# A second halved square per chunk, its low part as the third pass, T3 ahead of y, and the split of x1 shared with ScalarE

## The chip, the cores and the metric

The kernel runs on one core of one Trainium2 chip. The metric is the device time of one execution in microseconds. TensorE does matmuls, VectorE, ScalarE and GpSimd work elementwise, each with its own queue of instructions in a fixed order; semaphores tie the queues together. In profile rows they are PE (and PEld for its weight loads), DVE, ACT and POOL.

## The reference

```python
# attention over pooled keys, with k = v, then two MLPs, all fp32
kv_flat = kv.reshape(B, H//4, 4, W//4, 4, C).mean(axis=(2, 4)).reshape(B, -1, C) @ w_sr
a = softmax(q @ kv_flat.T / sqrt(C));  x = a @ kv_flat          # 12288 tokens x 128
x = (relu(x @ w_in1) ** 2) @ w_out1                             # d_ff 2048
h = x @ w_in2
P = a[0] + a[1]*h + a[2]*h**2 + a[3]*h**3
Q = 1 + |b[0]|*|h| + |b[1]|*h**2
out = (P / (Q + 1e-6)) @ w_out2
```

## The kernel before

Everything is kept transposed: 128 features on the partitions, tokens along the free dimension. Stage A (the first 300 us) is the attention and leaves X. Stage B, the other 1200 us, is both MLPs, in 24 chunks (NCH) of 512 tokens (T), each with 16 tiles of 128 hidden features (NF); 384 tiles (NB) in all.

Precision: an fp32 matmul is one instruction, shown as two records. Where a cheaper way is used, an operand is split into a rounded fp32r part ("h", high) and the rest ("l", low), and three fp32r passes (h.h, h.l, l.h) replace the fp32 matmul: in1 and in2, the first layers of both MLPs, always run so, through the helper three().

Each engine's program is a Python loop over steps s, unrolled; there is no planner. In step s:
- TensorE: in2(s - 19), then in1(s), then out2(s - 23), then out1(s - 2). in2 and in1 are the first layers, out2 and out1 the second ones, which add into one PSUM bank over the 16 tiles of a chunk. LAG = 19 is the distance of the second MLP behind the first.
- ScalarE, in this order: osb (the output copy of a finished chunk) in column 7, x2h and x2f (the high part and a full copy of the first MLP's result) in column 2, g1h (the high part of a halved square) and the square of tile s - 1 where it is ScalarE's, then for tile s - 19 the abs u and t1 = a3 h + a2 (tb), an hcb copy of h in column 10, ln of the denominator of tile s - 20, relu of tile s, and exp of tile s - 20, which gives r = 1/Q.
- GpSimd: in column 2 x2l = x2f - x2h; v = |b1| u + |b0| and w = v u of tile s - 19, with the T2 product of that tile between them in column 10 (T2_COL = 7, by_pool); then, if s is odd, the square of tile s, and g1l for a halved tile.
- VectorE: y = (t3 + a0) r of tile s - 21, T3 = (t2 + a1) h of tile s - 20, E (in place over r, from w) of tile s - 21, T2 = t1 h of tile s - 19, G2 of tile s - 21, the result that out2 reads.

"Column" here is s modulo 16. Squares of even tiles are ScalarE's, those of odd tiles GpSimd's; in chunk 0 ScalarE and VectorE make all of them. SPLIT_COLS = (13,) says which square of a chunk is "halved": ScalarE makes its high part g1h, GpSimd its low part g1l = g1 - g1h, and out1 runs three fp32r passes for that tile in place of one fp32 matmul.

Each chunk of X is split too, into x1h and x1l, by GpSimd: x1_high and x1_low in the loop from L388 on, in column 5 of the chunk before (chunks 2 to 23; the first two are split in stage A). in1 of the chunk's first tile waits for it (x1_rdy).

Rings: four PSUM banks for h (H2_RING), so in2(t) waits for G2 of tile t - 4; two for the first MLP (in1(t) waits for relu of tile t - 2). exp writes over h, so it waits for T3. out1 of a chunk's first tile waits for x2f of the chunk before, in2 of a chunk's first tile for x2l (L909). The DMA queue does nothing here but one output a chunk.

The only lines that order VectorE's work around the change are these:

```python
            for s in range(TAIL_S):
                t = s - LAG - 2      # y, waits r_rdy
...
                t = s - LAG - 1      # T3, waits t2_rdy or t2p_rdy
...
                t = s - LAG - 2      # E
...
                t = s - LAG          # T2, waits t1_rdy
...
                t = s - LAG - 2      # G2
```

Of the kernel before, what the change touches and what calls it, by code (L numbers as in the profile page):

```python
# [30 lines left out]
def build_program(nc, qT, kvT, w_sr, w_in1, w_out1, w_in2, w_out2, coef_a, coef_b, outT):  # L31
# [35 lines left out]
    with ExitStack() as ctx:  # L67
# [91 lines left out]
        sqh_rdy, sql_rdy = sem("sqh_rdy"), sem("sql_rdy")  # L159
        x2f_rdy, x2l0_rdy = sem("x2f_rdy"), sem("x2l0_rdy")  # L160
        wo1h_rdy, wo1_rdy, g1h_rdy, g1l_rdy = map(sem, ("wo1h_rdy", "wo1_rdy", "g1h_rdy", "g1l_rdy"))
        hc_rdy, t2p_rdy = sem("hc_rdy"), sem("t2p_rdy")
        o_out = [sem("o_out0"), sem("o_out1")]
        wout1_in = sem("wout1_in")
# [39 lines left out]

            return t < NF or t % 2 == 0

        SPLIT_COLS = (13,)

        def halved(t):

# [76 lines left out]
        def _(pool):  # L287
# [61 lines left out]

            def x1_low(c):  # L350

                pool.wait_ge(x1h_rdy, c + 1)
                nc.gpsimd.tensor_tensor(x1l[:, c % 2, :], X[:, c * T:(c + 1) * T], x1h[:, c % 2, :].bitcast(F32),
                                        ALU.subtract).then_inc(x1_rdy, 1)

# [30 lines left out]
            pool.wait_ge(babs_rdy, 1)  # L386

            for s in range(STEPS):  # L388
                if s % NF == 5 and 1 <= s // NF < NCH - 1:
                    x1_high(s // NF + 1)  # L390
                    x1_low(s // NF + 1)
                t = s - 3
                if chunk_end(t) and t > NF:
                    c = t // NF
                    pool.wait_ge(x2h_rdy, c + 1)
                    pool.wait_ge(x2f_rdy, c)
                    nc.gpsimd.tensor_tensor(x2l[:, c % 2, :], x2f[:, c % 2, :], x2h[:, c % 2, :].bitcast(F32),  # L397
                                            ALU.subtract).then_inc(x2_rdy, 1)
                t = s - LAG
                if in_b(t):  # L400
                    w = wb[:, t % W_RING, :]
                    u = ub[:, t % U_RING, :]
                    pool.wait_ge(u_rdy, t + 1)
                    nc.gpsimd.tensor_scalar(w, u, babs[:, 1:2], babs[:, 0:1], ALU.mult, ALU.add).then_inc(v_rdy, 1)  # L404
                    if by_pool(t):
                        n = pool_t2(t)
                        p = tb[:, t % T_RING, :]
                        pool.wait_ge(t1_rdy, t + 1)
                        pool.wait_ge(hc_rdy, n + 1)
                        nc.gpsimd.tensor_tensor(p, p, hcb[:, n % HC_RING, :], ALU.mult).then_inc(t2p_rdy, 1)  # L410
                    pool.wait_ge(v_rdy, t + 1)
                    nc.gpsimd.tensor_tensor(w, w, u, ALU.mult).then_inc(w_rdy, 1)  # L412
                t = s
                if in_b(t) and not on_act(t):
                    r = r1[:, t % R_RING, :]
                    pool.wait_ge(r1_rdy, t + 1)
                    need(pool, g1_used, t - G_RING + 1)
                    nc.gpsimd.tensor_tensor(g1[:, t % G_RING, :], r, r, ALU.mult).then_inc(sqp_rdy, 1)  # L418
                    if halved(t):
                        n = halves(t)  # L420
                        pool.wait_ge(sqh_rdy, n + 1)
                        pool.wait_ge(sqp_rdy, squares_pool(t))
                        nc.gpsimd.tensor_tensor(g1l[:, n % 2, :], g1[:, t % G_RING, :], g1h[:, n % 2, :].bitcast(F32),
                                                ALU.subtract).then_inc(sql_rdy, 1)
# [3 lines left out]
        def _(act):  # L428
# [78 lines left out]
            for s in range(STEPS):  # L507
# [35 lines left out]
                if s == NF + 1:  # L543
                    act.wait_ge(g1_used, NF)
                    nc.scalar.activation(x2h[:, 0, :], ACC1, ACT.Identity).then_inc(x2h_rdy, 1)

                t = s - LAG
                if in_b(t):
# [40 lines left out]
        def _(dve):  # L589
# [129 lines left out]
            dve.wait_ge(x2h_rdy, 1)  # L719
            nc.vector.tensor_tensor(x2l[:, 0, :], ACC1, x2h[:, 0, :].bitcast(F32), ALU.subtract).then_inc(x2l0_rdy, 1)  # L720

            for s in range(TAIL_S):
                t = s - LAG - 2
                if in_b(t):
                    y, r = tb[:, t % T_RING, :], h2(t)
                    dve.wait_ge(r_rdy, t + 1)
                    nc.vector.scalar_tensor_tensor(out=y, in0=y, scalar=ca[:, 0:1], in1=r,  # L727
                                                   op0=ALU.add, op1=ALU.mult).then_inc(y_rdy, 1)
                t = s - LAG - 1
                if in_b(t):  # L730
                    p = tb[:, t % T_RING, :]
                    if by_pool(t):
                        dve.wait_ge(t2p_rdy, pool_t2(t) + 1)
                    else:
                        dve.wait_ge(t2_rdy, t + 1 - pool_t2(t + 1))
                    nc.vector.scalar_tensor_tensor(out=p, in0=p, scalar=ca[:, 1:2], in1=h2(t),  # L736
                                                   op0=ALU.add, op1=ALU.mult).then_inc(t3_rdy, 1)
                t = s - LAG - 2
                if in_b(t):
                    r = h2(t)  # L740
                    nc.vector.scalar_tensor_tensor(out=r, in0=wb[:, t % W_RING, :], scalar=Q_ONE, in1=r,  # L741
                                                   op0=ALU.add, op1=ALU.mult).then_inc(e_rdy, 1)
                t = s - LAG
                if in_b(t) and not by_pool(t):
                    p = tb[:, t % T_RING, :]
                    dve.wait_ge(t1_rdy, t + 1)
                    nc.vector.tensor_tensor(p, p, h2(t), ALU.mult).then_inc(t2_rdy, 1)  # L747
                t = s - LAG - 2
                if in_b(t):
                    y = tb[:, t % T_RING, :]  # L750
                    dve.wait_ge(y_rdy, t + 1)
                    dve.wait_ge(e_rdy, t + 1)
                    nc.vector.scalar_tensor_tensor(out=y, in0=h2(t), scalar=-2.0, in1=y,  # L753
                                                   op0=ALU.add, op1=ALU.mult).then_inc(g2_rdy, 1)

            for s in range(TAIL_S, STEPS):
                t = s - LAG - 2
                if in_b(t):
                    y, r = tb[:, t % T_RING, :], h2(t)
                    dve.wait_ge(r_rdy, t + 1)  # L760
                    nc.vector.scalar_tensor_tensor(out=y, in0=y, scalar=ca[:, 0:1], in1=r,
                                                   op0=ALU.add, op1=ALU.mult).then_inc(y_rdy, 1)
                t = s - LAG - 1
                if in_b(t):
                    p = tb[:, t % T_RING, :]
                    if by_pool(t):
                        dve.wait_ge(t2p_rdy, pool_t2(t) + 1)
                    else:
                        dve.wait_ge(t2_rdy, t + 1 - pool_t2(t + 1))
                    nc.vector.scalar_tensor_tensor(out=p, in0=p, scalar=ca[:, 1:2], in1=h2(t),  # L770
                                                   op0=ALU.add, op1=ALU.mult).then_inc(t3_rdy, 1)
                t = s - LAG
                if in_b(t) and not by_pool(t):
                    p = tb[:, t % T_RING, :]
# [20 lines left out]
        def _(pe):  # L795
# [106 lines left out]
            def in2(t):  # L902

                if in_b(t):
                    c, f = t // NF, t % NF * P
                    if t == 0:
                        pe.wait_ge(wl_rdy, W_PARTS)
                    if t % NF == 0:
                        pe.wait_ge(*((x2l0_rdy, 1) if c == 0 else (x2_rdy, c)))  # L909
                    if t < WIDE + H2_RING:  # L910
                        need(pe, g2_rdy, t - H2_RING + 1)
                    elif t < WIDE + TAIL_RING:
                        pe.wait_ge(r1_rdy, NB)
                    else:
                        pe.wait_ge(g2_rdy, t - TAIL_RING + 1)
                    three(h2(t), win2h[:, f:f + P], win2l[:, f:f + P],
                          x2h[:, c % 2, :], x2l[:, c % 2, :]).then_inc(h2_rdy, 1)

            def in1(t):

# [26 lines left out]
            def out1(t):  # L947

                if in_b(t):
# [13 lines left out]
                    elif halved(t):  # L963
                        n = halves(t)
                        pe.wait_ge(sqh_rdy, n + 1)
                        pe.wait_ge(sql_rdy, n + 1)
                        three(ACC1, wo1h[:, f, :], wo1l[:, f, :], g1h[:, n % 2, :], g1l[:, n % 2, :],
                              start=(f == 0), stop=(f == NF - 1)).then_inc(g1_used, 1)
                    else:
                        if on_act(t):  # L970
                            pe.wait_ge(sqa_rdy, squares_act(t))
                        else:
                            pe.wait_ge(sqp_rdy, squares_pool(t))
                        mm(ACC1, wout1[:, f, :], g1[:, t % G_RING, :], start=(f == 0), stop=(f == NF - 1))\  # L974
                            .then_inc(g1_used, 1)
# [51 lines left out]
```

## Time and profile before

| | us |
|---|---|
| median of 3 runs | 1517.82 (1517.7 to 1518.0) |
| the profiled execution | 1517.89 |
| its span, first to last instruction | 1515.9 |
| TensorE busy | 1483.7 (98%) |
| VectorE busy | 1445.2 (95%) |
| ScalarE busy | 1378.8 (91%) |
| GpSimd busy | 1248.3 (82%) |

The granted clock of TensorE is 1.00 of full speed over the span. Busy times are unions of records, from an instruction's start to its end; since a next instruction may start before the last one's record ends, they say less than start times do. Matmul ends are modelled, and a matmul behind an fp32 one has its start shown early, so steps are best measured from the first x1h pass of a step (in1) to the next.

### The profile page before, as it was taken

To read this page: it belongs to the slowest core of one execution; us is meant where nothing else is said; L and a number is where in the kernel's file an instruction comes from. 1 tells how busy PE (TensorE), PEld (TensorE's weight loads), DVE (VectorE), ACT (ScalarE), POOL (GpSimd) and SP (SyncE) were. 2 spreads that over 40 slices of the span, in tenths; PEclk is the share of its full clock that TensorE was granted. 3 is DMA by queue.
4 is the path that set the end of the run, shared out by engine and by line. 5 is a ranking of instruction groups with operands and counts; after the bars stand their busy time and mean duration, and the time that the engine had idled before them with its cause. 6 is when DMAs were issued, how large, how long until landed. Compare 5 with 4: busy or idle time off the path is not lost.

```text
span 1515.9 us, 20584 instructions
## 1 busy us (share of the span) xinstructions
PE 1483.7 (98%) x5576; PEld 991.1 (65%) x5576; DVE 1445.2 (95%) x2549; ACT 1378.8 (91%) x2672; POOL 1248.3 (82%) x1225
## 2 busy tenths in 40 slices
PE   5999999999999999999999999999999999999988
PEld 4999999765666666666666666666666666666655
DVE  7888888889999999999999999999999999999998
ACT  3777777689999999999999999999999999999997
POOL 4544445359999999999999999999999999999897
PEclk9999999999999999999999999999999999999999
DMA  6200001000000000000000000000000000000000
GB/s 224 84 21 28 21 27 43 1 1 1 8 8 8 1 8 8 8 8 1 7 8 8 0 8 8 8 1 8 7 8 1 8 8 8 8 1 8 8 8 7
DMA packets 11518, 24.21 MB, mean 16 GB/s; under 512 B 1440, under 2 KB 2336, under 8 KB 11168
## 3 DMA queue, kind: packets, MB, share of 16 engines
q1 hardware_dynamic: 11424, 23.14, 4.5%
q8 instruction: 36, 0.59, 0.2%
q14 instruction: 58, 0.48, 0.1%
HBM read 16.85 MB, written 6.29 MB: 15 GB/s over the span
## 4 chain that ended last, share of the span: by engine, by line
PE 88%; DVE 5%; ACT 2%; POOL 2%; issue 1%; DMA 1%; SPq 0%; POOLq 0%; ACTq 0%; DVEq 0%
PE psum L937 19%; PE psum L974 18%; PE psum L801 11%; PE psum L800 11%; PE psum L802 11%; PE psum L889 6%; PE psum L852 6%; PE psum L874 4%; DVE tb L727 1%; DVE tb L736 1%; DVE tb L753 1%; DVE g1h L713 1%; DVE psum L741 1%; POOL tb L410 1%; DMA X<-kvT 1%
## 5 line engine op out<-in xcount | busy, mean ns | idle before, releaser
L412 POOL TENSOR_TENSOR wb<-wb,ub 128x512 f32<-128x512 f32 x384 | 496.4, 1293 | 29.4
L937 PE MATMUL psum<-tb,wout 128*128 128x512 f32 x736 | 375.8, 592 | 2.5 <-DVE tb L785 2.3
L974 PE MATMUL psum<-g,wout 128*128 128x512 f32 x690 | 352.4, 592 | 0.2 <-ACT x2f L528 0.2
L404 POOL TENSOR_SCALAR wb<-ub,babs 128x512 f32<-128x512 f32 x384 | 296.0, 771 | 35.5 <-ACT ub L550 30.3
L800 PE MATMUL psum<-x2h,win2h 128*128 128x512 f32 x384 | 283.3, 738 | 2.6 <-POOL x2l L397 2.5
L727 DVE SCALAR_TENSOR_TENSOR tb<-tb,ca,psum 128x512 f32<-128x512 f32 x364 | 267.8, 736 | 4.6 <-ACT psum L584 4.5
L736 DVE SCALAR_TENSOR_TENSOR tb<-tb,ca,psum 128x512 f32<-128x512 f32 x365 | 269.6, 739 | 0.0
L551 ACT ACTIVATE tb<-psum,ca 128x512 f32<-128x512 f32 x384 | 267.1, 696 | 0.0
L550 ACT ACTIVATE ub<-psum 128x512 f32<-128x512 f32 x384 | 233.0, 607 | 23.5 <-PE psum L802 23.5
L568 ACT ACTIVATE lnb<-wb 128x512 f32<-128x512 f32 x384 | 248.3, 647 | 5.2 <-POOL wb L412 4.8
L753 DVE SCALAR_TENSOR_TENSOR tb<-psum,tb 128x512 f32<-128x512 f32 x364 | 248.1, 682 | 2.6
L741 DVE SCALAR_TENSOR_TENSOR psum<-wb,psum 128x512 f32<-128x512 f32 x364 | 249.5, 685 | 0.0
L584 ACT ACTIVATE psum<-lnb 128x512 f32<-128x512 f32 x384 | 240.1, 625 | 2.6 <-DVE tb L770 0.6
L974 PEld LDWEIGHTS psum<-g,wout 128*128 128x128 f32 x690 | 130.9, 190 | 163.7 <-issue 162.0
L578 ACT ACTIVATE r<-psum 128x512 f32<-128x512 f32 x384 | 234.9, 612 | 2.4 <-PE psum L802 0.3
L747 DVE TENSOR_TENSOR tb<-tb,psum 128x512 f32<-128x512 f32 x343 | 232.5, 678 | 4.0 <-ACT tb L551 4.0
L418 POOL TENSOR_TENSOR g<-r 128x512 f32<-128x512 f32 x184 | 191.9, 1043 | 33.2 <-ACT r L578 33.2
L334 POOL TENSOR_SCALAR pnorm<-prob,stat 128x768 f32<-128x768 f32 x96 | 87.3, 909 | 127.8 <-DVE stat L637 122.0
L937 PEld LDWEIGHTS psum<-tb,wout 128*128 128x128 f32 x736 | 138.4, 188 | 36.4 <-DVE tb L785 3.8
L801 PE MATMUL psum<-x1l,win1h 128*128 128x512 f32 x384 | 153.0, 398 | 0.0
L801 PE MATMUL psum<-x2l,win2h 128*128 128x512 f32 x384 | 152.9, 398 | 0.0
L800 PE MATMUL psum<-x1h,win1h 128*128 128x512 f32 x384 | 151.9, 396 | 0.0
(109 smaller groups left out, 2506.6 us busy)
## 6 DMA issues: line engine op xcount, KB each, us to landing
qraw<-qT SPq DMA_DIRECT2D x23, 256.0 KB, 2.6
outT<-osb SPq DMA_DIRECT2D x23, 256.0 KB, 2.0
X<-kvT SPq DMA_DIRECT2D x15, 384.0 KB, 7.7
wraw<-w_in SPq DMA_DIRECT2D x2, 1024.0 KB, 8.3
X<-kvT SPq DMA_DIRECT2D x2, 192.0 KB, 10.5
outT<-osb SPq DMA_DIRECT2D x2, 128.0 KB, 1.8
qraw<-qT SPq DMA_DIRECT2D x1, 192.0 KB, 10.2
wsr<-w_sr SPq DMA_DIRECT2D x1, 64.0 KB, 1.8
```

Source lines behind the costliest of these rows:

```text
L404: nc.gpsimd.tensor_scalar(w, u, babs[:, 1:2], babs[:, 0:1], ALU.mult, ALU.add).then_inc(v_rdy, 1)
L412: nc.gpsimd.tensor_tensor(w, w, u, ALU.mult).then_inc(w_rdy, 1)
L551: nc.scalar.activation(tb[:, t % T_RING, :], h2(t), ACT.Identity, bias=ca[:, 2:3], scale=a3).then_inc(t1_rdy, 1)
L568: nc.scalar.activation(lnb[:, t % LN_RING, :], wb[:, t % W_RING, :], ACT.Ln, bias=Q_ONE).then_inc(ln_rdy, 1)
L727: nc.vector.scalar_tensor_tensor(out=y, in0=y, scalar=ca[:, 0:1], in1=r, op0=ALU.add, op1=ALU.mult).then_inc(y_rdy, 1)
L736: nc.vector.scalar_tensor_tensor(out=p, in0=p, scalar=ca[:, 1:2], in1=h2(t), op0=ALU.add, op1=ALU.mult).then_inc(t3_rdy, 1)
L741: nc.vector.scalar_tensor_tensor(out=r, in0=wb[:, t % W_RING, :], scalar=Q_ONE, in1=r, op0=ALU.add, op1=ALU.mult).then_inc(e_rdy, 1)
L753: nc.vector.scalar_tensor_tensor(out=y, in0=h2(t), scalar=-2.0, in1=y, op0=ALU.add, op1=ALU.mult).then_inc(g2_rdy, 1)
L800: mm(out, lh, rh, start=start, stop=False)
L801: mm(out, lh, rl, start=False, stop=False)
L937: mm(ACC2, wout2[:, f, :], tb[:, t % T_RING, :], start=(f == 0), stop=(f == NF - 1))\
L974: mm(ACC1, wout1[:, f, :], g1[:, t % G_RING, :], start=(f == 0), stop=(f == NF - 1))\
```

## The change

Four things:
- SPLIT_COLS is (5, 13): the square of tile 5 of each chunk from chunk 1 on is halved as well. ScalarE makes one more g1h (in column 6), GpSimd one more g1l (in column 5), TensorE three fp32r passes in place of an fp32 matmul.
- The order of passes in in2 and in out1 of halved tiles: the two passes that need the high part alone come first, and the wait for the low part stands only in front of the third. (In the code above L908 to L917 and L964 to L968.)
- VectorE's loop runs T3 (tile s - 20) before y (tile s - 21), except in steps whose T3 needs GpSimd's T2 product (column 11). In the steps from TAIL_S on the order is as before.
- x1's high part for chunks 2 to 23 is made by ScalarE in column 8, ahead of that step's abs; GpSimd's x1_low moves from column 5 to column 10, ahead of that step's v, and waits for the new semaphore.

```diff
-        SPLIT_COLS = (13,)
+        SPLIT_COLS = (5, 13)
...
             def x1_low(c):
-                pool.wait_ge(x1h_rdy, c + 1)
+                pool.wait_ge(*((x1h_rdy, c + 1) if c < 2 else (x1ha_rdy, c - 1)))
...
             for s in range(STEPS):
-                if s % NF == 5 and 1 <= s // NF < NCH - 1:
-                    x1_high(s // NF + 1)
+                if s % NF == 10 and 1 <= s // NF < NCH - 1:
                     x1_low(s // NF + 1)
...
+                if s % NF == 8 and 1 <= s // NF < NCH - 1:
+                    c = s // NF + 1
+                    act.wait_ge(x_rdy, c + 1)
+                    need(act, h1_rdy, (c - 1) * NF)
+                    nc.scalar.activation(x1h[:, c % 2, :], X[:, c * T:(c + 1) * T], ACT.Identity).then_inc(x1ha_rdy, 1)
...
+            for s in range(TAIL_S):
+                if by_pool(s - LAG - 1):
+                    make_y(s - LAG - 2)
+                    make_t3(s - LAG - 1)
+                else:
+                    make_t3(s - LAG - 1)
+                    make_y(s - LAG - 2)
...
                     if t % NF == 0:
-                        pe.wait_ge(*((x2l0_rdy, 1) if c == 0 else (x2_rdy, c)))
+                        pe.wait_ge(x2h_rdy, c + 1)
...
-                    three(h2(t), win2h[:, f:f + P], win2l[:, f:f + P],
-                          x2h[:, c % 2, :], x2l[:, c % 2, :]).then_inc(h2_rdy, 1)
+                    mm(h2(t), win2h[:, f:f + P], x2h[:, c % 2, :], start=True, stop=False)
+                    mm(h2(t), win2l[:, f:f + P], x2h[:, c % 2, :], start=False, stop=False)
+                    if t % NF == 0:
+                        pe.wait_ge(*((x2l0_rdy, 1) if c == 0 else (x2_rdy, c)))
+                    mm(h2(t), win2h[:, f:f + P], x2l[:, c % 2, :], start=False, stop=True).then_inc(h2_rdy, 1)
...
                         pe.wait_ge(sqh_rdy, n + 1)
+                        mm(ACC1, wo1h[:, f, :], g1h[:, n % 2, :], start=(f == 0), stop=False)
+                        mm(ACC1, wo1l[:, f, :], g1h[:, n % 2, :], start=False, stop=False)
                         pe.wait_ge(sql_rdy, n + 1)
-                        three(ACC1, wo1h[:, f, :], wo1l[:, f, :], g1h[:, n % 2, :], g1l[:, n % 2, :],
-                              start=(f == 0), stop=(f == NF - 1)).then_inc(g1_used, 1)
+                        mm(ACC1, wo1h[:, f, :], g1l[:, n % 2, :], start=False, stop=(f == NF - 1)).then_inc(g1_used, 1)
```

make_y and make_t3 hold the two instructions of the loop before, word for word.

## Rows read from the trace of the kernel before

**Rows 1.** The page: shares of the chain that ended last, by engine
```profile
PE 88%; DVE 5%; ACT 2%; POOL 2%; issue 1%; DMA 1%; SPq 0%; POOLq 0%; ACTq 0%; DVEq 0%
```

**Rows 2.** Windows: PE, PEld, DVE, ACT, POOL busy us, clock, DMA, GB/s
```profile
1000.00:1200.00 200.00, 200.00 (x649) 122.22 (x648) 198.81 (x320) 195.97 (x376) 187.11 (x182) 1.00 0.02 6
```

**Rows 3.** Timeline of PE: start us, us, line, op, out<-in; first x1h passes
```profile
703.78 0.39 PE L800 MATMUL psum<-x1h,win1h 128*128 128x512 f32 x1
...
706.73 0.40 PE L800 MATMUL psum<-x1h,win1h 128*128 128x512 f32 x1
...
756.38 0.40 PE L800 MATMUL psum<-x1h,win1h 128*128 128x512 f32 x1
```

**Rows 4.** Timeline of ACT in a stretch where it has a backlog
```profile
335.06 0.59 ACT L550 ACTIVATE ub<-psum 128x512 f32<-128x512 f32 x1
...
338.14 0.61 ACT L550 ACTIVATE ub<-psum 128x512 f32<-128x512 f32 x1
...
340.70 0.64 ACT L550 ACTIVATE ub<-psum 128x512 f32<-128x512 f32 x1
...
341.75 0.66 ACT L557 ACTIVATE hcb<-psum 128x512 f32<-128x512 f32 x1
342.23 0.70 ACT L568 ACTIVATE lnb<-wb 128x512 f32<-128x512 f32 x1
...
344.26 0.67 ACT L550 ACTIVATE ub<-psum 128x512 f32<-128x512 f32 x1
...
345.31 0.72 ACT L568 ACTIVATE lnb<-wb 128x512 f32<-128x512 f32 x1
```

**Rows 5.** Timeline of POOL, columns 5 and 9 to 10 of chunk 1
```profile
326.26 0.61 POOL L348 CAST x1h<-X 128x512 fp32r<-128x512 f32 x1
326.95 1.29 POOL L353 TENSOR_TENSOR x1l<-X,x1h 128x512 fp32r<-128x512 f32 x1
328.23 0.76 POOL L404 TENSOR_SCALAR wb<-ub,babs 128x512 f32<-128x512 f32 x1
...
338.85 0.77 POOL L404 TENSOR_SCALAR wb<-ub,babs 128x512 f32<-128x512 f32 x1
...
341.97 0.78 POOL L404 TENSOR_SCALAR wb<-ub,babs 128x512 f32<-128x512 f32 x1
342.70 1.29 POOL L410 TENSOR_TENSOR tb<-tb,hcb 128x512 f32<-128x512 f32 x1
343.95 1.28 POOL L412 TENSOR_TENSOR wb<-wb,ub 128x512 f32<-128x512 f32 x1
```

**Rows 6.** Timeline of DVE and PE at the first tile of the second MLP
```profile
318.52 0.69 DVE L720 TENSOR_TENSOR x2l<-psum,x2h 128x512 fp32r<-128x512 f32 x1 [1.68 <-ACT x2h L545]
...
319.66 0.40 PE L801 MATMUL psum<-x2l,win2h 128*128 128x512 f32 x1
```

**Rows 7.** Timeline of ACT, abs of column 13 and ln of column 15
```profile
797.06 0.60 ACT L550 ACTIVATE ub<-psum 128x512 f32<-128x512 f32 x1
...
804.47 0.63 ACT L568 ACTIVATE lnb<-wb 128x512 f32<-128x512 f32 x1
```

**Rows 8.** Timeline of ACT, last ln of column 11 and last abs of column 10
```profile
1388.18 0.66 ACT L568 ACTIVATE lnb<-wb 128x512 f32<-128x512 f32 x1
...
1433.21 0.60 ACT L550 ACTIVATE ub<-psum 128x512 f32<-128x512 f32 x1 [0.44 <-PE psum L802]
```

**Rows 9.** Timeline of DVE: T2, G2 and the next G2
```profile
764.95 0.68 DVE L747 TENSOR_TENSOR tb<-tb,psum 128x512 f32<-128x512 f32 x1
765.55 0.68 DVE L753 SCALAR_TENSOR_TENSOR tb<-psum,tb 128x512 f32<-128x512 f32 x1
...
768.66 0.68 DVE L753 SCALAR_TENSOR_TENSOR tb<-psum,tb 128x512 f32<-128x512 f32 x1
```

**Rows 10.** Waits: engine, line, waited for: us in total, times, longest
```profile
PEld psum L800 <- POOL x2l L397: 14.2, 23, 3.0
...
ACT lnb L568 <- POOL wb L412: 4.8, 8, 1.5
```

More of the change, by code:

```diff
@@ L161, in build_program @@
         wo1h_rdy, wo1_rdy, g1h_rdy, g1l_rdy = map(sem, ("wo1h_rdy", "wo1_rdy", "g1h_rdy", "g1l_rdy"))
+        x1ha_rdy = sem("x1ha_rdy")
         hc_rdy, t2p_rdy = sem("hc_rdy"), sem("t2p_rdy")
@@ L720, in _, with make_y @@
             nc.vector.tensor_tensor(x2l[:, 0, :], ACC1, x2h[:, 0, :].bitcast(F32), ALU.subtract).then_inc(x2l0_rdy, 1)
-            for s in range(TAIL_S):
-                t = s - LAG - 2
+            def make_y(t):
                 if in_b(t):
@@ L728, in _, with make_t3 @@
                                                    op0=ALU.add, op1=ALU.mult).then_inc(y_rdy, 1)
-                t = s - LAG - 1
+            def make_t3(t):
                 if in_b(t):
@@ L756, in _ @@
             for s in range(TAIL_S, STEPS):
[L757 to L771, printed above, removed]
+                make_y(s - LAG - 2)
+                make_t3(s - LAG - 1)
                 t = s - LAG
```

## The prediction

> **What bounds the kernel now.** I read the page's chain first: TensorE holds 88% of it [rows 1]. Then the windows: from 1000 to 1200 us TensorE 200.00 of 200 us, VectorE 198.8, ScalarE 196.0, GpSimd 187.1, granted clock 1.00 [rows 2]. Four engines are nearly full, so a share can't settle it; start-to-start times can. One chunk of 16 steps, from TensorE's first x1h pass to the same pass a chunk later, takes 756.38 - 706.73 = 49.65 us. The step with the halved square takes 706.73 - 703.78 = 2.95 us, the other fifteen (49.65 - 2.95) / 15 = 3.11 [rows 3]. The pass that is shorter by its own arithmetic makes a shorter step, which is how an engine looks that waits for nobody. The other engines hold slack: ScalarE's abs waits for TensorE's last pass of the tile (0.44 us idle in the row at 1433.21 [rows 8]).
>
> A share also hides this: an ACTIVATE record lasts 0.60 to 0.70 us, but when the engine has a backlog the next starts 0.48 to 0.57 us after the last. The stretch from 335.06 us shows that: abs to abs 3.08 us with a square, 2.56 us without (so 0.52 for a square), 3.56 us with a square and an hcb copy [rows 4]. So ScalarE's work per chunk is 16 x 2.56 + 8 squares x 0.52 + g1h 0.52 + hcb 0.48 (341.75 to 342.23) + x2h, x2f and osb, like copies out of PSUM, at the same 0.48 = 47.6 us of 49.65 [rows 4].
>
> Steps below are named by their number modulo 16 (column); the tile that runs the second MLP in step s is s - 19.
>
> **TensorE's side of the change.** A halved square costs TensorE three passes for one fp32 matmul: 3.11 - 2.95 = 0.16 us less a chunk [rows 3]. Column 5 adds one of them, so its own floor becomes 49.50. The order of the passes in in2 and in the halved out1 changes no count; it lets two passes (0.47 us) go before the low part is there. In the steady stretch TensorE has no stall to shorten; at the opening x2l is there at 319.21 and the first x2h pass really starts 0.23 before the next one's 319.66, so the third pass can go at about 319.57 in place of 319.90: 0.33 us [rows 6].
>
> **ScalarE's side.** Added per chunk: one g1h square and one x1h copy, both read from SBUF, each priced as the square from SBUF, 0.52 [rows 4]. No x1h copy runs on ScalarE in the trace; its bounds are 0.48 (hcb's spacing, from PSUM) and 0.72 (the whole record of ln at 345.31, which reads SBUF) [rows 4]. I take 0.52 since it too reads SBUF. ScalarE's work becomes 47.6 + 1.04 = 48.64, under 49.50. By sums alone the change fits. The Trainium skill (VectorE: DVE Perf Modes, section on the TRN2 errata) gives a ScalarE instruction from SBUF 224 + 512 cycles at 1.2 GHz, 613 ns; by it the copy would cost 0.09 us more a chunk and the total below 1.9 us more. The trace's spacing of 0.52 speaks against that.
>
> **GpSimd's side.** Removed: the x1h cast, 0.69 (326.26 to 326.95). Added: g1l at column 5, a like subtraction, 1.28. Moved: x1l, 1.28 (326.95 to 328.23, the row at 326.95 has 1.29), from column 5 to column 10 [rows 5]. Sum +0.6 on 187.11 / 200 x 49.65 = 46.4 [rows 2], again under 49.5. But column 10 is the column whose T2 product GpSimd makes (T2_COL = 7, and 7 + 19 = 26), and there x1l now stands in front of v, the product and w, and ScalarE's ln of the next step waits for w. GpSimd's queue from column 9, when it has a backlog, can be read in order: abs of column 9 at 338.14; v of column 9 at 338.85, then w and the square, v of column 10 at 341.97, product 342.70, w 343.95, ending at 345.23; ln at 345.31 [rows 4, 5]. From abs to w's end 7.09 us, with 0.03 for the semaphore 7.12. ScalarE itself needs from that abs to that ln 2.56 + 3.56 + 1.05 = 7.17. Today the two paths are level. With x1l in between, GpSimd's is 7.12 + 1.27 = 8.39: ln of column 11 comes 1.22 us late in each of the 22 chunks that split x1.
>
> Is that lateness paid for? It would be forgotten if ScalarE had 1.22 us of slack a chunk; it has 49.50 - 48.64 = 0.86. The loop that counts: ln of column 11, then ScalarE's own work to abs of column 9 in the next chunk (48.64 - 7.17), then GpSimd 8.39, back to ln. A second detour of this kind exists today: GpSimd's g1l between columns 13 and 15. Abs at 797.06, ln at 804.47, 7.41 us by GpSimd [rows 7]; ScalarE alone needs 3.08 (with g1h) + 3.08 + 1.05 = 7.21. That is 0.20, hidden today under 2 us of slack, and it lies on the same loop. At column 5 the new g1l makes none: to ln of column 7 ScalarE also has osb (0.48), so it needs 7.69 against 7.41. Removed with x1h and x1l at column 5 is a detour that cost nothing today. Loop: 48.64 + 1.22 + 0.20 = 50.06 us a chunk. TensorE (49.50) and VectorE (G2 to G2 3.11 a step, less one T2 of 0.60 a chunk: 49.2 [rows 9]) are faster, so the loop sets the pace, 0.40 above today's 49.66.
>
> **T3 in front of y** moves no work. T3 comes one instruction earlier, so exp may; y comes one later, a fifth of 3.11 or 0.6 us, which hides as much of exp's lateness. At column 11 the old order stays. VectorE isn't the bound, so I price it at zero. Without it the 1.2 us by which ln is late would reach y in column 12, and VectorE has 50.06 - 49.2 = 0.9 us a chunk to take that in: it is a cover, worth at most 0.3 us a chunk. It adds no wait: T3 waits for its own T2, one instruction back.
>
> **New waits and who is behind them.** x1l waits for x1ha two columns earlier: met. The copy on ScalarE stands in front of abs of column 8; that abs comes 0.5 later, within the loop's count. TensorE's x2l wait now has only the third pass behind it.
>
> **The sum**, against the profiled execution (1517.89 us, span 1515.9, 2.0 around it; the median of the three runs is 1517.82, the same).
> - First ln of column 11 (345.31 now [rows 4]): ScalarE has a backlog in that first stretch (the spacings of rows 4), so g1h and x1h count in full (+1.04), x1l adds 1.22, the opening gives back 0.33: +1.9.
> - 21 loops to the last one (1388.18 now [rows 8]): 21 x 50.06 = 1051.3 against 1388.18 - 345.31 = 1042.9: +8.4.
> - From there to abs of column 10 of the last chunk (1433.21 now, 45.03 us later [rows 8]) ScalarE needs 15 x 2.56 + 7 x 0.52 + 0.96 (x2h, x2f) + 0.52 + 0.48 + 0.20 - 1.05 = 43.1, and TensorE, which ran ahead, lets it: -1.9.
> - The last 83 us hold the drain, whose T2 products alternate between GpSimd and VectorE as before: 0.
> Together +8.4: **1517.89 + 8.4 = 1526.3 us**.
>
> **Rivals.**
> 1. It works as built (faster). The mechanism is the same loop, with a lateness that is absorbed: if x1l costs column 11 less than 0.66 us (50.06 - 49.50 = 0.56 off the sum of 1.42), TensorE sets the pace again. For it: x1l could overlap part of v, and GpSimd has 2 us of slack a chunk. Against it: every instruction of rows 5 starts where the last one ends. Price: 22 x 0.16 + 0.33 = 3.8 us less: 1514.0.
> 2. The detours don't add or are a little smaller, and the loop comes to 49.6 to 49.75: within 3 us of before, about 1518.5. If only the 0.20 of column 13 drops out, the loop is 49.86 and the time 1522.1, still slower; I count that to the forecast.
> 3. TensorE isn't the bound today, so its cheaper square gives nothing. The Trainium skill (Perfetto Trace Analysis, Identifying the Most-Contended Engine) calls matmul busy time a poor measure and judges headroom by weight loads. Weight loads take 122 of 200 us here and VectorE 198.8, so VectorE could be the bound [rows 2]: then chunks stay at 49.65 and the time at 1517.9. Against it: the 2.95 us step of rows 3, where VectorE's step is 3.11 [rows 9].
> 4. Larger losses: the x1h copy at its upper bound of 0.72 (21 x 0.20 = 4.2) or the 1.9 us at the end not recovered: 1530.5 and 1528.2.
>
> **How the numbers follow.** Forecast with its own range 1521 to 1530: 0.75. Rival 1: 0.13. Rivals 2 and 3: 0.10 together. Rival 4 beyond 1530: 0.02, the rest of it lies in the forecast's own range. The range goes from 1518.0, which takes in most of rival 2, to 1530.0. A measurement of this kernel tells about 0.2% (3 us) from no change. Faster by more: 0.13; within: 0.10; slower by more: 0.77.
>
> **What the profile would show.** Right: ln waits for GpSimd's w about 1.1 us once a chunk (the 1.22 less the 0.1 by which records overlap), some 24 us more than today's 4.8; TensorE idle about 0.5 us a chunk behind x2f or x2l, where today's 14.2 us of weight-load waits on x2l hold no matmul up [rows 10]; intervals between x1h passes over a chunk of 50.06, with ScalarE's abs late by over 1 us after column 11; x1h's spacing on ScalarE 0.52. Wrong: chunks of 49.50 with TensorE 100% busy and abs waiting for it (rival 1), or ln late but less than 0.7 us. The shape of the sum fails if waits other than ln's appear on ScalarE.

## The result, and the profile after

| | before | after |
|---|---|---|
| median, us | 1517.91 | 1535.39 |
| ratio | 1 | 1.0116 (95%: 1.0100 to 1.0131) |
| span of the profiled execution | 1515.9 | 1533.5 |
| ScalarE busy, 600 to 1400 us | 783.95 | 783.94 |

The change makes the kernel 17.5 us slower; 8.4 were forecast, so the time lies above the range of 1518 to 1530. The direction was right, the size wasn't.

The page of the changed kernel gives the shares of the chain that ended last, by engine, to be read against [rows 1]:

```profile
PE 71%; ACT 9%; POOL 8%; DVE 6%; issue 4%; DMA 1%; SPq 0%; POOLq 0%; ACTq 0%; DVEq 0%
```

TensorE's share fell from 88% to 71%; those of ScalarE and GpSimd rose from 2% each to 9% and 8%. The window of the steady stretch (columns as in [rows 2]) and four waits of the whole span (columns as in [rows 10], where ln's was 4.8):

```profile
600.00:1400.00 800.00, 794.37 (x2571) 481.09 (x2570) 785.24 (x1256) 783.94 (x1511) 747.31 (x714) 1.00 0.02 6
```

```profile
PEld psum L981 <- ACT x2f L528: 26.6, 22, 1.8
ACT lnb L574 <- POOL wb L412: 26.4, 29, 1.5
...
PE psum L981 <- ACT x2f L528: 8.4, 22, 1.0
...
PEld psum L943 <- ACT osb L514: 7.9, 22, 0.4
```

ln's wait for w rose to 26.4 us in total, near the forecast (4.8 + 24). TensorE now stands behind x2f once a chunk. Its timeline shows the first x1h pass of columns 0 to 3, and that of column 0 a chunk later:

```profile
964.27 0.40 PE L803 MATMUL psum<-x1h,win1h 128*128 128x512 f32 x1
...
967.38 0.39 PE L803 MATMUL psum<-x1h,win1h 128*128 128x512 f32 x1
...
970.50 0.39 PE L803 MATMUL psum<-x1h,win1h 128*128 128x512 f32 x1
...
972.55 1.12 PE L981 MATMUL psum<-g,wout 128*128 128x512 f32 x2 [0.33 <-ACT x2f L528]
...
974.31 0.39 PE L803 MATMUL psum<-x1h,win1h 128*128 128x512 f32 x1
...
1014.71 0.40 PE L803 MATMUL psum<-x1h,win1h 128*128 128x512 f32 x1
```

A chunk takes 1014.71 - 964.27 = 50.44 us (49.65 before [rows 3]); the step in which out1 waits for x2f takes 3.81 instead of 3.11. The new halved square's own saving doesn't show either: its step, from 986.79 to 989.91, takes 3.12 and not 2.95, since TensorE waits there for ScalarE's osb (last row of the waits above). What makes ScalarE late stands seven columns ahead of the wait at x2f. Here is ScalarE from abs of column 9 to ln of column 11, then GpSimd in the same stretch; [rows 4] and [rows 5] show the like for the kernel before:

```profile
943.50 0.83 ACT L556 ACTIVATE ub<-psum 128x512 f32<-128x512 f32 x1
...
946.06 0.86 ACT L556 ACTIVATE ub<-psum 128x512 f32<-128x512 f32 x1
...
949.66 0.86 ACT L556 ACTIVATE ub<-psum 128x512 f32<-128x512 f32 x1
950.14 0.96 ACT L557 ACTIVATE tb<-psum,ca 128x512 f32<-128x512 f32 x1
952.09 0.64 ACT L574 ACTIVATE lnb<-wb 128x512 f32<-128x512 f32 x1 [0.99 <-POOL wb L412]
```

```profile
944.43 0.77 POOL L404 TENSOR_SCALAR wb<-ub,babs 128x512 f32<-128x512 f32 x1 [0.91 <-ACT ub L556]
945.28 1.30 POOL L412 TENSOR_TENSOR wb<-wb,ub 128x512 f32<-128x512 f32 x1
946.54 1.04 POOL L418 TENSOR_TENSOR g<-r 128x512 f32<-128x512 f32 x1
947.54 1.28 POOL L354 TENSOR_TENSOR x1l<-X,x1h 128x512 fp32r<-128x512 f32 x1
948.80 0.78 POOL L404 TENSOR_SCALAR wb<-ub,babs 128x512 f32<-128x512 f32 x1
949.54 1.28 POOL L410 TENSOR_TENSOR tb<-tb,hcb 128x512 f32<-128x512 f32 x1
950.77 1.28 POOL L412 TENSOR_TENSOR wb<-wb,ub 128x512 f32<-128x512 f32 x1
```

GpSimd runs seven instructions without a gap, x1l in the middle of them. w ends at 952.05 and ln starts at 952.09. That is 1.95 us after t1 started; elsewhere ln follows t1 after 0.57, so it is 1.38 late. ScalarE's busy share is the same before and after: this loss doesn't show in a share.

### The profile page after: what moved, and what is told of

Same layout as the page of the kernel before. It is cut to its first block, busy times and chain, and to the rows that moved or that the text cites. A ratio compares the mean times of both kernels' runs of the same rounds, so it can differ in the third digit from the quotient of the medians.

```text
span 1533.5 us, 20699 instructions
## 1 busy us (share of the span) xinstructions
PE 1493.7 (97%) x5599; PEld 990.8 (65%) x5599; DVE 1447.7 (94%) x2549; ACT 1395.3 (91%) x2717; POOL 1265.5 (83%) x1226
## 4 chain that ended last, share of the span: by engine, by line
PE 71%; ACT 9%; POOL 8%; DVE 6%; issue 4%; DMA 1%; SPq 0%; POOLq 0%; ACTq 0%; DVEq 0%
PE psum L943 14%; PE psum L981 14%; PE psum L892 6%; PE psum L855 6%; PE psum L923 4%; PE psum L920 4%; PE psum L919 4%; PE psum L804 4%; PE psum L803 4%; PE psum L877 4%; PE psum L805 4%; POOL wb L412 3%; ACT psum L590 3%; ACT ub L556 1%; POOL wb L404 1%
## 5 line engine op out<-in xcount | busy, mean ns | idle before, releaser
L981 PE MATMUL psum<-g,wout 128*128 128x512 f32 x644 | 331.1, 596 | 8.4 <-ACT x2f L528 8.4
L557 ACT ACTIVATE tb<-psum,ca 128x512 f32<-128x512 f32 x384 | 307.7, 801 | 0.0
L574 ACT ACTIVATE lnb<-wb 128x512 f32<-128x512 f32 x384 | 280.7, 731 | 27.9 <-POOL wb L412 26.4
L744 DVE SCALAR_TENSOR_TENSOR tb<-tb,ca,psum 128x512 f32<-128x512 f32 x384 | 281.9, 734 | 13.1 <-POOL tb L410 13.0
L733 DVE SCALAR_TENSOR_TENSOR tb<-tb,ca,psum 128x512 f32<-128x512 f32 x384 | 283.1, 737 | 7.9 <-ACT psum L590 7.7
L919 PE MATMUL psum<-x2h,win2h 128*128 128x512 f32 x384 | 278.5, 725 | 0.9 <-DVE tb L769 0.7
L590 ACT ACTIVATE psum<-lnb 128x512 f32<-128x512 f32 x384 | 271.6, 707 | 2.6 <-DVE tb L744 0.6
L556 ACT ACTIVATE ub<-psum 128x512 f32<-128x512 f32 x384 | 268.8, 700 | 2.2 <-PE psum L923 2.0
L584 ACT ACTIVATE r<-psum 128x512 f32<-128x512 f32 x384 | 267.2, 696 | 2.4 <-PE psum L805 0.3
L981 PEld LDWEIGHTS psum<-g,wout 128*128 128x128 f32 x644 | 120.4, 190 | 168.3 <-issue 140.8
L920 PE MATMUL psum<-x2h,win2l 128*128 128x512 f32 x384 | 152.7, 398 | 0.0
```

Source lines behind the costliest of these rows:

```text
L556: nc.scalar.activation(ub[:, t % U_RING, :], h2(t), ACT.Abs).then_inc(u_rdy, 1)
L557: nc.scalar.activation(tb[:, t % T_RING, :], h2(t), ACT.Identity, bias=ca[:, 2:3], scale=a3).then_inc(t1_rdy, 1)
L574: nc.scalar.activation(lnb[:, t % LN_RING, :], wb[:, t % W_RING, :], ACT.Ln, bias=Q_ONE).then_inc(ln_rdy, 1)
L584: nc.scalar.activation(r1[:, t % R_RING, :], H1[t % H1_RING], ACT.Relu).then_inc(r1_rdy, 1)
L590: nc.scalar.activation(h2(t), lnb[:, t % LN_RING, :], ACT.Exp, scale=-1.0).then_inc(r_rdy, 1)
L919: mm(h2(t), win2h[:, f:f + P], x2h[:, c % 2, :], start=True, stop=False)
```

## The experiments

Theory A is the prediction's: the pace is set by a loop of ScalarE's own work and of the places where GpSimd's queue makes ln late ("detours"). Rivals: ScalarE is overloaded wherever x1l stands; the new order of passes or of T3 and y holds something up. P is the time of a chunk in the steady stretch. The medians of before in the three groups of runs are 1518.03, 1517.77 and 1517.93 us.

**x1l in column 8**

```diff
-                if s % NF == 10 and 1 <= s // NF < NCH - 1:
+                if s % NF == 8 and 1 <= s // NF < NCH - 1:
                     x1_low(s // NF + 1)
```

> The changed kernel with GpSimd's x1l in column 8 in place of column 10, everything else as changed. Theory A (a loop of ScalarE's work plus GpSimd's detours sets the pace): in column 8 ScalarE has x1h of its own in front of abs, so from abs of column 7 to ln of column 9 it needs 7.2 us against GpSimd's 7.3; the 1.4 us wait of ln in column 11 goes, the loop falls to about 49.1, TensorE sets the pace again at 49.50 us a chunk: 1514 to 1515 us. Theory B (ScalarE is simply overloaded by its two new instructions, wherever x1l stands): stays at 1535. Theory C (TensorE is held up by the new order of passes): stays at 1535.

Measured: 1515.26 us, ratio 0.9981 (0.9972 to 0.9990). One GpSimd instruction moved by two columns gives back 20 us. Its chunk, from TensorE's timeline, and its windows:

```profile
755.15 0.40 PE L803 MATMUL psum<-x1h,win1h 128*128 128x512 f32 x1
...
804.65 0.40 PE L803 MATMUL psum<-x1h,win1h 128*128 128x512 f32 x1
```

```profile
600.00:1400.00 800.00, 800.00 (x2622) 494.27 (x2621) 797.81 (x1278) 798.69 (x1537) 761.63 (x728) 1.00 0.02 6
```

P = 49.50, TensorE's new floor, as priced; both halved squares now have steps of 2.95, and TensorE is busy for 800.00 of 800. Theory A holds. The overload theory falls, for ScalarE does the same instructions here, and so does the one by which the new order of passes holds something up, for it is the same too. This is the fastest version of the study, 2.8 us under the kernel before.

**x1l in column 10, but behind w; and x1l in column 12**

```diff
-                if s % NF == 10 and 1 <= s // NF < NCH - 1:
-                    x1_low(s // NF + 1)
...
                     nc.gpsimd.tensor_tensor(w, w, u, ALU.mult).then_inc(w_rdy, 1)
+                if s % NF == 10 and 1 <= s // NF < NCH - 1:
+                    x1_low(s // NF + 1)
```

> The changed kernel with GpSimd's x1l in column 10, but behind that step's w in place of in front of v. Theory A: the w that ln of column 11 waits for is no longer delayed, but that of column 11 is, by x1l; GpSimd needs 10.6 us from abs of column 9 to ln of column 12, ScalarE 9.75: 0.8 us late in place of 1.4. Loop 48.65 + 0.8 + 0.25 + 0.1 = 49.85, so about 1523. Theory B: 1535.

> The changed kernel with x1l in column 12. If only the steps next to x1l count, GpSimd is 0.56 us late there plus 0.25 in column 15 and TensorE nearly sets the pace: 1516. If, as the run with x1l behind w suggests (1532, not 1523), GpSimd's whole queue from column 9 to column 15 counts, the same instructions stand in it and the loop stays at 50.2: 1531 to 1532.

Measured: 1531.95 us (P 50.23) and 1531.52 us (P 50.27). The 1523 expected of the first was a miss. I had followed GpSimd's queue only to the next ln. In these runs ln is late in several columns (0.16 in column 11, 0.78 in 12, 0.52 in 15 with x1l behind w; 0.17, 0.82 in column 13 and 0.52 with x1l in column 12), with much the same sum of 1.5 us, against 1.39 + 0.25 in the changed kernel. From column 9 to column 15 GpSimd hardly idles, so it doesn't matter where in that stretch the 1.27 us stand; ahead of it GpSimd waits for abs of column 9 (0.91 us idle in the row at 944.43), and there most of them is absorbed: with x1l in column 8, ln of columns 9, 11 and 15 is 0.05, 0.24 and 0.22 late.

**One halved square a chunk**

```diff
-        SPLIT_COLS = (5, 13)
+        SPLIT_COLS = (13,)
```

> The changed kernel with one halved square a chunk (column 13 alone), everything else as changed. Theory A: TensorE's floor rises by 0.16 to 49.66, but ScalarE loses one instruction of 0.52, so the loop falls from 50.42 to 49.90: about 1524, faster than the changed kernel by 11 us although TensorE has more to do. If TensorE set the pace, it would be 3.4 us slower than the changed kernel: 1539.

Measured: 1524.74 us, ratio 1.0045 (1.0029 to 1.0060), P 49.95. TensorE has 0.16 us a chunk more to do than in the changed kernel, and the kernel is 10.7 us faster: TensorE doesn't set the pace of the changed kernel. The edit takes two instructions out of each chunk, ScalarE's g1h (0.52) and GpSimd's g1l. P falls by 0.47, near the 0.52; ln was late in columns 11 and 15 alone, where this g1l doesn't stand. In this run abs waits for TensorE in columns 6 and 10 (0.25 and 0.14 us a chunk), so TensorE is near the path again.

**VectorE's old order**

```diff
-                if by_pool(s - LAG - 1):
+                if True:
                     make_y(s - LAG - 2)
```

> The changed kernel with VectorE's old order everywhere (y in front of T3). Theory A: VectorE isn't in the loop; it must now take in exp's lateness in y, 0.9 us a chunk less than it needs at most 0.3: 1535 to 1541. If the new order is what costs, it falls toward 1518.

Measured: 1535.82 us, P 50.42. T3 ahead of y neither costs nor gains anything here.

**The second halved square alone**

```diff
# on the kernel before
-        SPLIT_COLS = (13,)
+        SPLIT_COLS = (5, 13)
```

> The kernel before with nothing but the second halved square (column 5); x1h and x1l stay on GpSimd in column 5. TensorE alone: 49.50 a chunk, 1514.5. By the loop: ScalarE's work 47.6 + 0.52 = 48.13, GpSimd's queue from abs of column 3 to ln of column 7 (with x1h, x1l, g1l) 14.6 us against ScalarE's 13.4, 1.2 late, and 0.25 in column 15, 0.2 for records that lengthen: 49.8, so about 1521.

Measured: 1525.21 us, ratio 1.0048 (1.0032 to 1.0063), P 49.97, where 1521 and 49.8 were expected. Without moving x1h and x1l out of column 5 the halved square costs 7 us: they and g1l are then in one stretch of GpSimd's queue, and ln of column 7 is 1.0 late. So its gain has to come with another place for x1's split: with x1l in column 8 the two halved squares gain, with x1l in column 10 they lose.

**An additional GpSimd instruction**, first on the kernel before

```diff
+                if s % NF == 10 and 1 <= s // NF < NCH - 1:
+                    nc.gpsimd.tensor_tensor(wraw[:, 0:T], X[:, 0:T], X[:, T:2 * T], ALU.subtract)
```

> The kernel before with an additional GpSimd subtraction (1.27 us, its result unused) in column 10 ahead of v, in each of the 22 chunks: the same delay of w as x1l makes in the changed kernel, but with ScalarE's work at 47.6. Theory A: the loop is 47.6 + 1.2 + 0.2 + 0.3 = 49.3, still under TensorE's 49.65: no change, 1518. If x1l's place costs by itself, whatever ScalarE's slack: up to 16 us more, 1534.

Measured: 1526.10 us, ratio 1.0054 (1.0039 to 1.0070). P is 50.08 in the profiled execution, which at 1527.78 us was the longest of the four, 1.7 above their median; a usual one has a P nearer 50.0. Theory A as I had summed it said no change. ScalarE's timeline in one chunk of this run shows its idle times in columns 6, 10 and 11:

```profile
829.64 0.60 ACT L552 ACTIVATE ub<-psum 128x512 f32<-128x512 f32 x1 [0.44 <-PE psum L804]
...
842.12 0.60 ACT L552 ACTIVATE ub<-psum 128x512 f32<-128x512 f32 x1 [0.29 <-PE psum L804]
...
847.52 0.64 ACT L570 ACTIVATE lnb<-wb 128x512 f32<-128x512 f32 x1 [0.63 <-POOL wb L414]
```

Two abs wait for TensorE here, so I asked whether the loop runs through TensorE, whose step at x2l takes 3.50 us in this run in place of 3.11. The new order of passes lets it go ahead of x2l:

```diff
# on before_extra10: in2 and the halved out1 as in the changed kernel
+                    mm(h2(t), win2h[:, f:f + P], x2h[:, c % 2, :], start=True, stop=False)
+                    mm(h2(t), win2l[:, f:f + P], x2h[:, c % 2, :], start=False, stop=False)
+                    if t % NF == 0:
+                        pe.wait_ge(*((x2l0_rdy, 1) if c == 0 else (x2_rdy, c)))
```

> The run before_extra10 (1526.1: kernel before plus one GpSimd subtraction in column 10) with the new order of passes. There TensorE stands 0.37 us a chunk at the chunk's first in2 behind x2l, and ScalarE waits for TensorE in columns 4, 6 and 10: the loop seems to run through TensorE. If so, two passes ahead of the wait (0.47 us) open it: 50.08 falls to 49.65 or 49.7, 1518 to 1519. If the loop is ScalarE and GpSimd alone: 1526.

Measured: 1525.88 us, P 50.01. TensorE no longer stands at in2 but 0.3 us a chunk at out2 behind osb, and nothing is gained: that guess falls too. What I had left out is the detour that the prediction dismissed: x1h and x1l in column 5. By the starts of [rows 5], from abs of column 3 to w of column 5 GpSimd needs 10.05 us, ScalarE to the same ln 9.27: 0.78 late. The idle times agree: in column 6 abs waits 0.53 longer than its turn and ln 0.21 (together 0.74), in 10 and 11 0.44 and 0.78 (1.22). With 0.23 in column 15 the detours add up to 2.2 us, and 47.6 + 2.2 is 49.8. The rest of the way is the subject of the next section.

**The same on the changed kernel**, behind x1l:

```diff
                     x1_low(s // NF + 1)
+                    nc.gpsimd.tensor_tensor(wraw[:, 0:T], X[:, 0:T], X[:, T:2 * T], ALU.subtract)
```

> The changed kernel with one more GpSimd subtraction (1.27 us, result unused) in column 10 behind x1l, in 22 chunks. Theory A: it lies wholly in the loop, 21 to 22 x 1.27 = 27 us more: 1562. If GpSimd's lateness were partly absorbed, clearly less.

Measured: 1561.43 us, P 51.65, 26.0 us more for 22 instructions of 1.27, 28 us if all counted: GpSimd's time in this place goes into the end nearly one for one.

**The old order of passes**, on the changed kernel and on the one with x1l in column 8:

```diff
-                    mm(h2(t), win2h[:, f:f + P], x2h[:, c % 2, :], start=True, stop=False)
...
+                    three(h2(t), win2h[:, f:f + P], win2l[:, f:f + P],
+                          x2h[:, c % 2, :], x2l[:, c % 2, :]).then_inc(h2_rdy, 1)
```

> The changed kernel with the old order of passes in in2 and halved out1, x1l left in column 10. Theory A: TensorE waits 0.7 us a chunk for ScalarE anyway and isn't in the loop: 1535.4, within 1 us. If the order of passes feeds the loop (TensorE held at a chunk's first tile by x2l, 0.4 us sooner than needed), up to 0.3 us a chunk more: 1541.

> The run with x1l in column 8 (1515.3), with the old order of passes in in2 and out1 (low part second, one wait in front of all three). If the order of passes does nothing once TensorE sets the pace: 1515.3, plus up to 0.3 for the opening. If x2l is late by more than before, because ScalarE's x2h and x2f come later in column 2: up to 0.2 us a chunk more, 1519.

Measured: 1535.16 us (P 50.41) and 1515.61 us (P 49.49, beside 1515.26). The order of passes is worth nothing that these medians can tell: 0.35 us for it in one pair, 0.23 against it in the other. The prediction gave it 0.33 at the opening; in the traces the new order has the first ln of column 11 earlier by 0.60 us (347.03 against 347.63) and by 1.00 with x1l in column 8 (346.13 against 347.13).

**A third halved square**, on x1l in column 8

```diff
-        SPLIT_COLS = (5, 13)
+        SPLIT_COLS = (5, 7, 13)
```

> The run x1l_col8 (1515.3) with a third halved square, in column 7. TensorE's floor 49.34. ScalarE's work 49.17; GpSimd's queue from column 7 on gets 1.27 us more with x1l in it, about 1 us late, plus 0.25 in column 15 and 0.3 for lengthening records: loop about 50.6, 1538. By TensorE alone 1512.

Measured: 1544.91 us, P 50.84. Expected 1538; the way is right, and the loop is longer again than by my sum. TensorE's floor of 49.34 isn't reached: each halved square buys it 0.16 us with 0.52 of ScalarE's and 1.27 of GpSimd's, and here ln of column 9 is 1.13 late.

## Why the prediction was right and wrong

**What bounds before**: right. TensorE sets the pace, and with x1l out of the way it does so again at 49.49 to 49.50, the floor priced at 49.50. The rival by which TensorE isn't the bound would have left the run with x1l in column 8 at 49.65.

**The mechanism**: right. ln of column 11 late behind w in each chunk, TensorE idle behind x2f, an x1h copy on ScalarE at 0.52 (its next instruction starts 0.52 or 0.53 later in all 22 cases), T3 and, in the steady stretch, the order of passes at nothing.

**The sum**: 8.4 against 17.6 us of span. First ln of column 11: +1.7 (347.03 against 345.31), forecast +1.9. The 21 loops: (1405.93 - 347.03) / 21 = 50.42 us each, forecast 50.06; 21 x 0.36 = 7.6 us of the miss. From there to abs of column 10 (1450.22): -0.7, forecast -1.9; the last stretch +0.6, forecast 0. Of the 1.2 us missing in front of abs of column 10, 0.52 is a slip of the sum: it counts one g1h, and the trace has two there, in columns 6 and 14. Another 0.42 is that abs itself, which starts that much later than its turn; in the kernel before it waits for TensorE [rows 8]. What the last stretch holds no run looked into.

**The step that failed** is "ScalarE's work 48.64 + detours 1.42", a loop of 50.06 where 50.42 was measured. Here are its terms by ScalarE's start times in a chunk. The instructions at their mean spacing sum to 48.73: the 2.56 us of a step, read to 0.01 and taken 16 times, is 2.57. ln of column 11 is 1.39 late (priced 1.22) and ln of column 15 0.25 (0.20); 0.05 is in small pieces. So 0.17 of the missing 0.36 us is at ln of column 11. Why is it later than by the rows of before? GpSimd's part is as priced, 7.62 from v at 944.43 to w's end, against 6.38 + 1.27 by [rows 5]; the semaphore's 0.03, which no row showed, is 0.04 here (952.05 to 952.09). But abs of column 9, whose end starts that part, takes 0.83 us where I had used the row of 0.61 at 338.14 [rows 4]. ScalarE's abs instructions in one unbroken run of the changed kernel:

```profile
965.71 0.59 ACT L556 ACTIVATE ub<-psum 128x512 f32<-128x512 f32 x1
...
975.41 0.68 ACT L556 ACTIVATE ub<-psum 128x512 f32<-128x512 f32 x1
...
984.15 0.76 ACT L556 ACTIVATE ub<-psum 128x512 f32<-128x512 f32 x1
...
993.89 0.84 ACT L556 ACTIVATE ub<-psum 128x512 f32<-128x512 f32 x1
996.46 0.87 ACT L556 ACTIVATE ub<-psum 128x512 f32<-128x512 f32 x1
```

Over ten steps the record grows from 0.59 to 0.87, 28 ns a step (about 23 over the three steps from 953.63, 0.59, to 962.89, 0.66): the start runs ahead of the end. After a wait it is 0.6 again. So what waits for the end of an abs comes later than the spacing of starts, on which my whole ScalarE sum stood, lets it. It was to be seen in [rows 4]: 0.59, 0.61, 0.64, 0.67 for the same instruction.

The same shortfall is in the other runs. With a constant 0.37 added the sum comes out at 50.43 for the changed kernel (50.42 measured), 49.91 for one halved square (49.95), 51.70 with the additional GpSimd instruction (51.65) and about 49.9 for the second halved square alone (49.97); without it all four are 0.3 to 0.4 short. The constant is 16 steps at 23 ns; at 28 ns it would be 0.45. Since the growth was seen before it was chosen, and rounding explains 0.09 of the shortfall by itself, these fits show that something of this size is missing in each run, not that it is the growth. The run with the old order of passes speaks for work rather than a delay that one could take away. There abs of column 4 starts 0.1 us later than its turn, the records start afresh, abs of column 9 takes 0.66 and ln of column 11 waits less,

```profile
843.31 0.66 ACT L556 ACTIVATE ub<-psum 128x512 f32<-128x512 f32 x1
...
849.45 0.72 ACT L556 ACTIVATE ub<-psum 128x512 f32<-128x512 f32 x1
...
851.72 0.63 ACT L574 ACTIVATE lnb<-wb 128x512 f32<-128x512 f32 x1 [0.98 <-POOL wb L412]
```

851.72 - 843.31 = 8.41 in place of 952.09 - 943.50 = 8.59, and P is the same 50.41. But from column 4 to 6 of that run abs follows abs after 3.11 and 3.12 us, which is TensorE's step (ScalarE's own is 3.09), so TensorE may have its part in this P. That abs of column 9 is 0.2 us longer than priced, and ln of column 11 as much later, is measured. That growing records account for the rest of the 0.36 is argued; no run changed the growth by itself, and why starts run ahead stays open.

**Two smaller faults**, which did no harm to the number but would to the next one. "At column 5 a detour that cost nothing today" was true of the kernel before alone; before_extra10 shows that it adds to the others as soon as the sum passes TensorE's floor. And a detour was followed only to the next ln, where a queue that stays full carries it on (x1l behind w).

**The chances**: 0.77 on slower was right; the range was too narrow, because its upper end took its costs from single rows and had none for the sum of spacings itself.

## What to carry to other kernels

When several engines are nearly full, look for the loop: one engine's work over a period plus each place where another engine's queue makes it late, and compare the sum with the pace, since detours that are free one by one add up. An instruction handed to a lightly loaded engine belongs where that engine idles, not where it has least to do by count: here two columns decided between +1.2% and -0.2%. Check in a full stretch whether records of one kind grow along it; where they do, price what waits for their ends from the late, long records.

## What the runs showed of the hardware

- ScalarE with a backlog: starts 0.48 us apart behind an instruction that reads 512 columns out of PSUM (0.57 behind t1) and 0.52 behind one that reads SBUF, with abs records of 0.59 us growing to 0.87 over ten steps and no further (there single spacings of 0.49 and 0.54 appear). After one spacing that is 0.1 us longer they are short again. The Trainium skill (VectorE: DVE Perf Modes, section on the TRN2 errata) puts 224 + 512 cycles, 613 ns, on the SBUF case. The record of ln right after a wait, 0.63 to 0.64, is near that; the spacing is not: the 22 copies of x1 start their successor after 0.52 or 0.53.
- GpSimd's 512-column subtraction of two tensors took 1.25 to 1.30 us start to start as x1l, in each of columns 5, 8, 10 and 12.
- ScalarE's busy share was 783.95 of 800 us before and 783.94 after, though its work grew by two instructions a chunk and its pace fell by 1.6%.
